# Sinks as fp32r products over 128 rows, routing logits from weights held on four column strips

## What is computed

```python
B, H, S, D = 4, 8, 768, 64; n_sink, window = 4, 128
keep = (key < n_sink) | (0 <= query - key < window)
a = softmax(where(keep, q @ k.T / sqrt(D), -1e9)); x = (a @ v) as rows [3072, 512]
do = x @ w_skip > 0                                    # tokens that an expert takes
logits = x @ w_gate; e = argmax(logits)                # 8 experts
x[do] += softmax(logits)[e] * (relu(x @ w1[e]) @ w2[e])
out = (relu(x @ w_in) ** 2) @ w_out                    # 512 -> 2048 -> 512
```

## Time and profile before

| | us |
|---|---|
| median of 3 runs | 1014.6 |
| the profiled execution, its own time | 1012.09 |
| its span | 1010.5 |
| PE busy | 974.5 (96%) |
| DVE busy | 444.7 (44%) |
| ACT busy | 406.7 (40%) |
| attention stage, to the last tile's logits | 213.15 |

### The profile page before, as it was taken

The page is one execution under the profiler, slowest core; times in us unless marked ns, Lnnn a source line. Parts: engine busy times, 40 slices in busy tenths (PEclk is TensorE's granted clock), DMA queues, the critical chain, the costliest instruction groups (busy, mean ns, idle before and its releaser), DMA issues.

```text
span 1010.5 us, 16431 instructions
## 1 busy us (share of the span) xinstructions
PE 974.5 (96%) x5432; PEld 788.1 (78%) x5433; DVE 444.7 (44%) x1343; ACT 406.7 (40%) x953; POOL 62.7 (6%) x106
## 2 busy tenths in 40 slices
PE   7999999949999999969999999999999999999997
PEld 5888787837888888857888888888888888888886
DVE  5777788755455555526323222322322232232223
ACT  6777788715555555515213212212221231222122
POOL 2111111120111111110000000000000000000000
PEclk9999999978999999989999999999999999999999
DMA  5445655377366666641002000200010020002001
GB/s 173 149 151 172 200 202 163 122 249 228 100 224 238 224 228 218 221 182 42 0 1 84 1 1 1 83 0 0 19 64 0 0 83 0 0 0 83 0 0 42
DMA packets 41632, 99.73 MB, mean 99 GB/s; under 512 B 6141, under 2 KB 6141, under 8 KB 41584
## 3 DMA queue, kind: packets, MB, share of 16 engines
q1 hardware_dynamic: 35712, 86.54, 25.0%
q0 software_dynamic: 4720, 10.69, 3.0%
q10 hardware_dynamic: 1152, 1.90, 0.5%
HBM read 78.24 MB, written 25.82 MB: 103 GB/s over the span
## 4 chain that ended last, share of the span: by engine, by line
PE 95%; DMA 2%; DVE 1%; ACT 1%; issue 1%; SPq 0%; DVEq 0%; POOLq 0%; ACTq 0%
PE bank L919 27%; PE bank L933 27%; PE bank L842 10%; PE bank L861 9%; PE bank L714 5%; PE bank L740 4%; PE bank L767 4%; PE bank L760 2%; PE bank L789 2%; PE bank L850 1%; PE bank L778 1%; PE bank L901 1%; PE bank L834 1%; ACT prob L564 1%; PE bank L725 0%
## 5 line engine op out<-in xcount | busy, mean ns | idle before, releaser
L1209 DVE TENSOR_TENSOR g<-relu_c 128x512 f32<-128x512 f32 x96 | 66.5, 693 | 362.7 <-ACT relu_c L660 362.6
L660 ACT ACTIVATE relu_c<-bank 128x512 f32<-128x512 f32 x96 | 57.6, 600 | 386.4 <-PE bank L919 386.4
L933 PE MATMUL bank<-w_hi,g_lo 128*128 128x512 f32 x384 | 153.0, 399 | 0.0
L919 PE MATMUL bank<-x_hi,w_lo 128*128 128x512 f32 x384 | 151.7, 395 | 0.9 <-DVE x_lo L1202 0.9
L919 PE MATMUL bank<-x_hi,w_hi 128*128 128x512 f32 x384 | 152.1, 396 | 0.0
L933 PE MATMUL bank<-w_hi,g_hi 128*128 128x512 f32 x384 | 152.0, 396 | 0.0
L919 PE MATMUL bank<-x_lo,w_hi 128*128 128x512 f32 x384 | 151.8, 395 | 0.0
L933 PE MATMUL bank<-w_lo,g_hi 128*128 128x512 f32 x384 | 151.8, 395 | 0.0
L305 DVE TENSOR_TENSOR w_lo<-w_raw,w_hi 128x1024 fp32r<-128x1024 f32 x80 | 94.5, 1215 | 10.1 <-ACT w_hi L300 10.1
L564 ACT ACTIVATE prob<-score,neg_max 128x264 f32<-128x264 f32 (+1 forms) x192 | 92.6, 485 | 3.0 <-DVE neg_max L992 3.0
L919 PEld LDWEIGHTS bank<-x_hi,w_lo 128*128 128x128 f32 x384 | 72.1, 188 | 18.8 <-issue 1.2
(11 more groups left out here) (126 smaller groups left out, 1324.8 us busy)
## 6 DMA issues: line engine op xcount, KB each, us to landing
w_raw<-in_weights SPq DMA_DIRECT2D x80, 512.0 KB, 5.3
x_c<-x_rows SPq DMA_DIRECT2D x28, 256.0 KB, 3.4
k_in<-in_kT SPq DMA_DIRECT2D x24, 264.0 KB
q_in<-in_qT SPq DMA_DIRECT2D x24, 256.0 KB, 3.0
v_in<-in_v SPq DMA_DIRECT2D x24, 256.0 KB, 3.0
x_rows<-x_row SPq DMA_DIRECT2D x24, 256.0 KB, 2.8
out<-w_raw SPq DMA_DIRECT2D x12, 512.0 KB, 2.9
x_raw<-routed SPq DMA_DIRECT2D x19, 260.0 KB, 3.1
```

The costliest lines, as they stand in the source:

```text
L919: ins = eng.matmul(hc_ps[f % 2][:, :], w[f // UNIT][:, f % UNIT, wcols], x[:, c, :], start=(c == 0 and n == 0), stop=(c == DC - 1 and n == 2))
L933: ins = eng.matmul(yc_ps[s][:, :], gg[:, f % 2, s * P:(s + 1) * P], w[f // UNIT][:, f % UNIT, DM:CH], start=(f == 0 and n == 0), stop=(f = ...
L1209: eng.tensor_tensor(g[:, f % 2, :], relu_c[:, f % 2, :], relu_c[:, f % 2, :], ALU.mult).then_inc(s_cg, 1)
```

## The change

Sinks: POOL writes `prob_sink` in four groups of 32 columns: the probabilities rounded to fp32r, what the rounding left off, and both once more. One transpose of 128 columns, one copy of [128, 128]. The 128 rows of v for the sinks (`vs_in`, four copies in DRAM) become `vs_part`: ACT rounds all of them to fp32r (`upper_sinks`, once per batch), and DVE puts into rows 64 to 127 what rounding left off (`lower_sinks`). The four products are fp32r matmuls over 128 rows: high by high, low by high, high by low, low by low.

Logits: four matmuls with `w_r` (now padded to 32 columns per pair) stationary, one on each strip of 32 columns of PE, and `xT_a` moved; they write the second 128 columns of `turn_ps[0]` and stand before the transpose of the sinks. ACT copies them to `lgT`, PE transposes `lgT` back after `turn(i,1)` (`logits_back`), and DVE reads `head_logit` from that.

```diff
@@ vs_in, parts
-        vs_in = sb("vs_in", [H * NS, 2, DM], F32, big)
+        vs_in = sb("vs_in", [P, 2, DM], F32, big)
+        vs_part = sb("vs_part", [P, 2, DM], F32R, big)
...
@@ SP, load_sinks
-                    eng.wait_ge(s_pv, ITEMS * NT * (b - 1))
+                    eng.wait_ge(s_vspart, b - 1)
@@ POOL
-                    eng.tensor_copy(prob_sink[:, :, :], prob[:, i % 2, :, KB * own_at(i):KB * own_at(i) + NS]).then_inc(s_psink, 1)
+                    sinks = prob[:, i % 2, :, KB * own_at(i):KB * own_at(i) + NS].rearrange("p (v h) k -> p v h k", v=1).to_broadcast([P, 2, H, NS])
+                    eng.tensor_copy(prob_sink[:, :, 0, :, :], sinks).then_inc(s_pshi, 1)
+                    eng.wait_ge(s_pshi, i + 1)
+                    eng.tensor_tensor(prob_sink[:, :, 1, :, :], sinks, prob_sink[:, :, 0, :, :].bitcast(F32), ALU.subtract).then_inc(s_psink, 1)
@@ ACT
+            def upper_sinks(b):
...
+                eng.activation(vs_part[:, b % 2, :], vs_in[:, b % 2, :], ACT.Copy).then_inc(s_vshi, 1)
...
+                if i == 1:
+                    upper_sinks(0)
...
                 if a:
                     exps(i, (4, 5))
+                if c:
+                    eng.wait_ge(s_lgT, i - 1)
+                    if bb:
+                        eng.wait_ge(s_turn, ITEMS * i)
+                    if i >= 3:
+                        eng.wait_ge(s_logit, i - 2)
+                    eng.activation(lgT[:, :], turn_ps[0][:, P:2 * P], ACT.Copy).then_inc(s_lgturned, 1)
                 if bb:
                     turned(i - 1, SINK)
...
+                if a and i % NT == NT - 2 and i // NT + 1 < B:
+                    upper_sinks(i // NT + 1)
@@ PE, product of the sinks
-                        ins = eng.matmul(oT_ps[:, p * P:(p + 1) * P], vs_in[:, b % 2, p * P:(p + 1) * P], sinkT[:, :],
+                        ins = eng.matmul(oT_ps[:, p * P:(p + 1) * P], vs_part[:, b % 2, p * P:(p + 1) * P], sinkT[:, :],
@@ PE, logits
-                for p in range(PAIRS):
-                    ins = eng.matmul(route_ps[:, 2 * p * LOGITS:2 * (p + 1) * LOGITS], xT_a[:, p, :], w_r[:, p, :], start=True, stop=True)
-                ins.then_inc(s_logit, 1)
+                eng.wait_ge(s_xT, i + 1)
+                eng.wait_ge(s_turned, ITEMS * (i + 1) + 3 if i + 1 < TILES else ITEMS * (i + 1))
+                for p in range(PAIRS):
+                    ins = eng.matmul(turn_ps[0][p * LG:(p + 1) * LG, P:2 * P], w_r[:, p, :], xT_a[:, p, :], start=True, stop=True)
+                ins.then_inc(s_lgT, 1)
+            def logits_back(i):
+                eng.wait_ge(s_lgturned, i + 1)
+                if i >= 1:
+                    eng.wait_ge(s_top, i)
+                eng.transpose(route_ps[:, 0:P], lgT[:, :], ident[:, :]).then_inc(s_logit, 1)
@@ DVE
+            def lower_sinks(b):
+                eng.wait_ge(s_vshi, b + 1)
+                lo = slice(P // 2, P)
+                eng.tensor_tensor(vs_part[lo, b % 2, :], vs_in[lo, b % 2, :], vs_part[lo, b % 2, :].bitcast(F32), ALU.subtract).then_inc(s_vspart, 1)
...
                 if bb:
                     reciprocals(i - 1)
+                if i == 1:
+                    lower_sinks(0)
+                if a and i % NT == NT - 1 and i // NT + 1 < B:
+                    lower_sinks(i // NT + 1)
```

More of the change, by code:

```diff
@@ L39 @@
 LOGITS = 1 + E
+LG = P // (H // 2)
 MAX_TILES = N // P + 2 * E
@@ L72, in build @@
     assert window == P and 0 < NS and H * NS <= P, "a window of one tile; the sinks of all heads in one"
+    assert 4 * H * NS == P and 2 * LOGITS <= LG, "sinks in high and low parts fill the rows; logits of a pair in its columns"
     KB = NS + P
@@ L99, in build @@
         v_in = sb("v_in", [P, RING, DM], F32, big)
-        vs_in = sb("vs_in", [H * NS, 2, DM], F32, big)
+        vs_in = sb("vs_in", [P, 2, DM], F32, big)
+        vs_part = sb("vs_part", [P, 2, DM], F32R, big)
         score = sb("score", [P, 2, H, 2 * KB], F32, big)
         prob = sb("prob", [P, 2, H, 2 * KB], F32, big)
-        prob_sink = sb("prob_sink", [P, H, NS], F32, big)
+        prob_sink = sb("prob_sink", [P, 2, 2, H, NS], F32R, big)
         probT = sb("probT", [P, PAIRS, 4 * P], F32, big)
-        sinkT = sb("sinkT", [H * NS, P], F32, big)
+        sinkT = sb("sinkT", [P, P], F32R, big)
+        lgT = sb("lgT", [P, P], F32, big)
         big.close()
@@ L130, in build @@
         xT_a = sbr("xT_a", [P, PAIRS, P], F32)
-        w_r = sbr("w_r", [P, PAIRS, 2 * LOGITS], F32)
+        w_r = sbr("w_r", [P, PAIRS, LG], F32)
         token_id = sbr("token_id", [P, TILES], I32)
@@ L193, in build @@
         s_vs = [sem(f"s_vs{n}") for n in range(2)]
+        s_vshi, s_vspart, s_pshi = sem("s_vshi"), sem("s_vspart"), sem("s_pshi")
+        s_lgT, s_lgturned = sem("s_lgT"), sem("s_lgturned")
         s_score, s_max, s_exp, s_psink = sem("s_score"), sem("s_max"), sem("s_exp"), sem("s_psink")
@@ L573, in turned @@
                 if k == SINK:
-                    eng.activation(sinkT[:, :], turn_ps[0][0:H * NS, 0:P], ACT.Copy).then_inc(s_turned, 1)
+                    eng.activation(sinkT[:, :], turn_ps[0][:, 0:P], ACT.Copy).then_inc(s_turned, 1)
                 else:
@@ L577, in turned @@
                     eng.activation(probT[:, k, 0:cols], turn_ps[k % 2][:, 0:cols], ACT.Copy).then_inc(s_turned, 1)
+            def upper_sinks(b):
+                eng.wait_ge(s_vs[b % 2], 16 * (b // 2 + 1))
+                if b >= 2:
+                    eng.wait_ge(s_pv, ITEMS * NT * (b - 1))
+                eng.activation(vs_part[:, b % 2, :], vs_in[:, b % 2, :], ACT.Copy).then_inc(s_vshi, 1)
             for i in range(TILES + 3):
                 a, bb, c, d = step_flags(i)
+                if i == 1:
+                    upper_sinks(0)
                 if d:
@@ L724, in turn @@
                     eng.wait_ge(s_psink, i + 1)
-                    ins = eng.transpose(to[0:H * NS, 0:P], prob_sink[:, :, :].rearrange("p h k -> p (h k)"), ident[:, :])
+                    ins = eng.transpose(to[:, 0:P], prob_sink[:, :, :, :, :].bitcast(F32).rearrange("p v s h k -> p (v s h k)"), ident[:, :])
                 else:
@@ L810, in _ @@
                     product(i - 1, 1)
+                if c:
+                    logits(i - 2)
+                if bb:
                     turn(i - 1, SINK)
@@ L815, in _ @@
                     rows_back(i - 2)
-                    logits(i - 2)
                 if a:
@@ L819, in _ @@
                     turn(i, 1)
+                if c:
+                    logits_back(i - 2)
                 if i + 1 < TILES:
@@ L999, in heads @@
                     eng.wait_ge(s_logit, j + 1)
-                    return eng.tensor_tensor(head_logit[:, :, :], route_ps[:, 0:H * LOGITS].rearrange("p (h c) -> p h c", h=H),
-                                             recip[:, j % 2, :].rearrange("p (h o) -> p h o", o=1).to_broadcast([P, H, LOGITS]), ALU.mult)
+                    pairs = route_ps[:, 0:P].rearrange("p (a c) -> p a c", a=PAIRS)[:, :, 0:2 * LOGITS]
+                    return eng.tensor_tensor(head_logit[:, :, :].rearrange("p (a b) c -> p a b c", b=2), pairs.rearrange("p a (b c) -> p a b c", b=2),
+                                             recip[:, j % 2, :].rearrange("p (a b o) -> p a b o", b=2, o=1).to_broadcast([P, PAIRS, 2, LOGITS]), ALU.mult)
                 def total():
@@ L1261 @@
         vs[:, h, :, h, :] = v[:, h, :ns, :]
-    vs = vs.reshape(B, H * ns, DM)
+    vs = np.broadcast_to(vs.reshape(B, 1, H * ns, DM), (B, 4, H * ns, DM)).reshape(B, 4 * H * ns, DM)
     wr = np.concatenate([moe_w_skip[:, None], moe_w_gate], axis=1).reshape(PAIRS, 2, D, LOGITS)
-    w_route = np.zeros((2, D, PAIRS, 2, LOGITS), wr.dtype)
+    w_route = np.zeros((2, D, PAIRS, LG), wr.dtype)
     for half in range(2):
-        w_route[half, :, :, half, :] = wr[:, half].transpose(1, 0, 2)
-    w_route = w_route.reshape(P, PAIRS, 2 * LOGITS)
+        w_route[half, :, :, half * LOGITS:(half + 1) * LOGITS] = wr[:, half].transpose(1, 0, 2)
+    w_route = w_route.reshape(P, PAIRS, LG)
     experts = np.concatenate([moe_w1.reshape(E, DC, P, F).transpose(0, 2, 1, 3),
```

5 lines of the change are left out of this document (2 added, 3 removed).

## The result

| | before | after |
|---|---|---|
| median of 13 runs each, on the same chip, us | 1013.31 | 1016.07 |
| ratio after/before, 95% interval | | 1.0025 [1.0013, 1.0036] |
| span of the profiled execution, us | 1010.5 | 1014.9 |
| PE busy | 974.5 (96%) | 959.5 (95%) |
| last tile's `ranks` on PE | 215.59 | 218.10 |

What follows compares the result with a forecast made beforehand. A ring over ACT and DVE, 8.48 us rising to 8.77, was taken to bound the changed kernel. Terms 0.9 + 0.4 + 0.2 - 0.3 - 1.1 - 1.5 = -1.4, so 1014.6 + 1.4 = 1016.0 us, range 1013.0 to 1021.0.

Steps and rivals of the forecast that it cites:

- The ring of 8.48: Attention stage: waits closing over ACT and DVE from one `turn(i,0)` to the next, 8.48 us, 0.32 under PE's 8.80.
- 0.125 and 0.16: Additions to the ACT and DVE waits: 0.125 for the transpose back, 0.16 for the copy to `lgT`, giving 8.77.
- four strips then buy no more than two: Logits on PE: matmuls on the same strip queue one behind the other, so 0.51 us instead of 0.80.
- already the ring's time: Step of 8.62 at a one-block tile, said to be bound by ACT and DVE; 0.16 longer, two lose 0.3.
- The two full steps of 9.04: Full steps after a one-block tile in the kernel before: DVE's chunk decided there; gain 0.1 each.
- Step 17: One-block step; `lower_sinks`, chunk's lower part and routing delay the maximum to T0 + 2.2, `upper_sinks` on ACT: loss 1.1 us.
- The end: Last tiles' serial work: `rows_back` waits behind logits of 0.51; 0.55 for each of two tiles, 0.4 before: loss 1.5 us.
- this ring as a rival: `rows_back`, x_row, `turn(i,1)` decide if fp32r gains nothing (chance 0.18): 8.95 to 9.07 per step, 6 to 8 us slower.
- fp32r at the fp32 price: Rival: sinks' product over 128 columns costs 0.95 to 1.08; slower, 1021 to 1023, with cheap strips 1017 to 1019; chance 0.18.
- strips one after another: Rival: logits on PE cost 1.08; 8.5 us slower, 1023; chance 0.06.
- copies that don't overlap: Rival: `lgT` on ACT costs 0.25, step 8.86; slower by 3.0, 1017.6; chance 0.15.
- That PE stays the bound: Rival: 0.81 kept in some 20 steps, 16 us faster, 998, or half of it, 1006; chance 0.10.

Runs made afterwards that it cites:

- four spare copies: Kernel before, plus four unread 128x128 ACT copies ahead of the copy to `sinkT` in each step: ratio 1.0104, 10.5 us slower, full step 9.27.
- with `expl` later: Kernel before, the routing's exponential moved on ACT behind the first two exponentials and pair 2's copy: ratio 0.9994; same move on the changed kernel: 0.9996.
- The low halves early: Changed kernel, DVE making the low halves of the sinks before normalising x_row: ratio 1.0012 to before, 1.2 us slower; step 17 is 8.46 instead of 9.33.
- The logits' half alone: Kernel before with only the change's logits part, sinks kept in fp32 on 32 rows: ratio 1.0051, 5.2 us slower, full step 9.10.
- the last two kernels: Sinks part only, and both parts reordered, each with `expl` moved back and low halves made earlier: ratios to before 0.9907 and 0.9901, 9.4 and 10.0 us faster.
- the sinks' half: Kernel before with only the change's sinks part, logits and their place as before: ratio 0.9969, 3.1 us faster, full step 8.61.
- the new arrangement of the logits: Both parts; `rows_back` before the sinks' transpose, logits behind ranks into bank 7, `lgT` copy behind `sinkT`, `expl` and low halves moved: ratio 0.9901, step 8.14.
- the single spare copy: Kernel before, plus one unread 128x128 ACT copy ahead of the copy to `sinkT` in each step: ratio 1.0006, full step 8.80.
- the sinks' half with the low halves early: Only the change's sinks part, DVE making the low halves before normalising x_row: ratio to before 0.9947, 5.4 us faster, full step 8.61.

## Why the prediction was right, and where it was not

**The bound and the period.** The ring of 8.48 was read from the rows of before, and four spare copies measured it as 8.48. With 0.125 and 0.16 the forecast had 8.77 a step; 8.77 came, with the wait where it was foretold. That it agrees to the last digit is luck, since its parts are off by up to 0.03, some up and some down. The forecast holds on its main point: 0.81 of PE's time were worth 0.03.

**The result by the numbers.** Forecast 1.4 slower, measured 2.5 (1.3 to 3.6). That 1016.0 and 1016.07 agree so closely is partly chance: before was at 1014.6 in the runs shown and at 1013.3 in these. I put 0.45 on "within 0.2%" and as much on "slower"; it is at 0.25%, with an interval from 0.13 to 0.36, so that the runs don't decide between the two. The sum came out near by misses of both signs: the table above has them, from 0.6 too little at the one-block tiles to 0.3 too much at the end.

**The sizes on PE.** Both sat inside their bounds and off the first ring, so they cost the forecast nothing in full steps. The sinks' product is 0.50, not 0.43: four matmuls of 128 rows and 128 columns in fp32r at 0.125 each, what a transpose takes, where I had the weight side of the logits (0.10). Its transpose takes 64.17 to 64.34 = 0.17, where 32 columns took 0.12; I had put the difference at nothing. The logits are 0.36, not 0.51: the step "four strips then buy no more than two" failed. By the Trainium skill (TensorE: Matmul & The Clock Gate, Part 3, Measured speedup vs the span model) packed tiles run together, a few ns apart; the estimate from that rule was about 0.28. The measured 0.36 decides: it is 0.08 above the rule's and 0.15 below my row's. PE's work came to 7.96 (8.77 less the 0.81 in front of T0, with `rows_back` at 0.47 by the starts of the earlier trace rows), against 7.99.

**The copies.** `lgT` 0.15: right. `expl` 2.11 behind the maximum: right. `head_logit` hidden: right, DVE still waits 0.20 for the scores.

**The second ring.** That 8.62 is "already the ring's time" was wrong in its name. It is the ring over the copy of pair 3, `rows_back` and the logits. The change takes the logits out of it, and the first ring, 8.77, came in its place: this loss of 0.15 is as forecast, by luck. But I charged only two steps, with 0.3; five steps around the one-block tiles lose 0.11 to 0.42 each, 0.93 in all, the largest miss of the sum. The largest of them (7.54 before, 7.96 after) has its waits on PE's timeline of the changed kernel, x_row's among them, which I had left out here:

```profile
100.30 0.41 PE L768 MATMUL bank<-ident,prob 128*128 128x128 f32 x2 [0.37 <-DVE x_row L1132]
...
105.52 0.66 PE L795 MATMUL bank<-probT,v_in 128*64 128x128 f32 x8 [0.44 <-ACT probT L586]
```

The two full steps of 9.04, where I said that DVE's chunk decided, were read wrongly. In the kernel before, DVE's first chunk starts at 126.17, behind the first of these steps, which ends at 124.55. In both, `rows_back` stands 0.25 later behind the ranks than elsewhere, which is the second ring; with `expl` later they are 8.80, the chunk in the second one notwithstanding. In the changed kernel they are 8.83 and 8.77, but the step behind the first of them is 9.05.

**Step 17.** Right in place and in what is late; 1.66 instead of 1.1. The first maximum comes 2.67 behind T0 (151.61 to 154.28) and not 2.2, which is most of the miss. The low halves early took back 0.87.

**The end.** 1.5 forecast, 1.18 measured. The forecast charged 0.51 for the logits in front of `rows_back` twice; at 0.36 its own sum would be 1.2.

**x_row.** The delay from x_row to PE was taken as the instruction's own 0.69; with the way to PE it is 0.84. In the full steps of the change this had no effect, because the first ring was longer. It decided the case with `expl` moved, and my expectation of 7 to 9 us fell with it. The price of this ring as a rival was off as well: the prediction lets it pass 8.77 once sinks and logits cost over 1.2 together, and by that 1.46 to 1.59 would give 9.03 to 9.16, not the 8.95 to 9.07 stated. The logits' half alone has 1.08 + 0.36 = 1.44 and a step of 9.10, at 5.2 us (3.6 to 6.7) where the rival was put at 6 to 8.

**Rivals.** fp32r at the fp32 price, strips one after another, and copies that don't overlap are ruled out by the rows. That PE stays the bound is false for the change; the last two kernels, which move what waits, come close to it.

## What to carry to other kernels

Where the chain of waits shows one engine without a break, sum every ring that closes over the other engines before a saving on it is priced: copies, waits for the routing, and the delay from one engine to the next. The slack is cheap to measure: put spare instructions into the ring until the period moves; the period less the time that they add is the ring's length. Once the bound has moved, look for the instruction that waits in a queue while others behind it are ready; with the sinks' half, moving `expl` and one DVE instruction was worth 6.3 us by the ratios, while the new arrangement of the logits added 0.6, which the intervals can't tell from nothing.

## What the runs showed that was not expected

- Four strips side by side: 8 records in 0.36, 0.045 each, against 0.064 for the products on two halves (16 in 1.02), and 0.10 for the old logits.
- An ACT copy of 128 columns costs its queue 0.15 as `lgT`, read from PSUM and lasting 0.26, and 0.20 as a spare copy, read from `ident` in SBUF and lasting 0.30. It is 0.20 for the single spare copy too (57.46 to 57.66 in that run's ACT timeline), so it isn't that four stand in a row; whether the source makes the difference was not tested.
- In the profile of the sinks' half alone the granted clock fell to 0.62 and 0.69 over ten microseconds; the transposes and scores there took twice their time, so 1.2 GHz. The product ahead of it had waited 0.70 us for xT_a; the changed kernel (at 158.30) and the sinks' half with the low halves early (at 154.87) wait as long at the same instruction, and their clock stayed at 1.00 there. That gap alone doesn't explain it, and what does was not found. By their mean granted clock, 0.979, two of the eleven unprofiled runs probably have it too. PE's timeline, sinks' half alone:

```profile
155.06 0.66 PE L786 MATMUL bank<-probT,v_in 128*64 128x128 f32 x8 [0.70 <-DVE xT_a L1120]
...
158.60 1.95 PE L759 MATMUL bank<-ident,prob 128*128 128x128 f32 x8
```
